# Weight parts of a fused attention and feed-forward kernel arrive where their low halves will stand, two per turn

## What is computed

```python
def _attn_ref(q, k, v, p):                  # q,k,v: 8 batches, 8 heads, 576 x 64; p: 32 x 64 per head
    p_packed = sm_attn(p, k, v)             # softmax(p k^T / 8) v
    return sm_attn(q, p_packed, p_packed)   # softmax(q pp^T / 8) pp

def _moe_ref(x, w_in, w_out, a, b):         # w_in 512 x 2048, w_out 2048 x 512
    h = x @ w_in
    P = a[0] + a[1] * h + a[2] * h * h + a[3] * h * h * h
    Q = 1.0 + np.abs(b[0]) * np.abs(h) + np.abs(b[1]) * h * h
    return (P / (Q + 1e-06)) @ w_out

def _moe2_ref(x, w_in, w_out, g_ln):        # 512 -> 1024 -> 512, softmax-weighted h, layer norm
    ...
```

## Time and profile before

| | us |
|---|---|
| median of 3 runs | 1235.49 |
| lowest and highest | 1233.49, 1236.66 |
| the profiled execution, its own time | 1235.92 |
| its span (first to last instruction) | 1234.1 |
| TensorE busy | 1180.6 (96%) |
| VectorE busy | 1045.4 (85%) |
| ScalarE busy | 832.8 (67%) |
| GpSimd busy | 437.5 (35%) |

### The profile page before, as it was taken

How to read it: one execution, slowest core, us unless ns; L and a number is a source line. 1 busy time by engine, 2 the same in 40 slices (tenths; PEclk the granted TensorE clock), 3 DMA queues, 4 the chain that set the end, 5 groups by cost and what they waited for, 6 DMA issues and landing times.

```text
span 1234.1 us, 25214 instructions
## 1 busy us (share of the span) xinstructions
PE 1180.6 (96%) x9824; PEld 1049.5 (85%) x9824; DVE 1045.4 (85%) x1621; ACT 832.8 (67%) x1302; POOL 437.5 (35%) x284
## 2 busy tenths in 40 slices
PE   6788887999999999999999999999999999999998
PEld 3455555999999999999999999997788888888887
DVE  3767778999999999999999999988677687776763
ACT  2456559888888888888888888754555454454543
POOL 1333322334343343333433334354434344353300
PEclk8889889999999999999999999999999999999999
DMA  8779975321202212012121121121121121111211
GB/s 286 226 265 348 333 272 217 105 81 38 81 28 64 81 38 80 29 62 81 43 75 37 55 80 37 54 88 44 43 54 49 36 58 43 51 47 38 60 26 35
DMA packets 70758, 116.25 MB, mean 94 GB/s; under 512 B 9728, under 2 KB 40448, under 8 KB 70656
## 3 DMA queue, kind: packets, MB, share of 16 engines
q1 hardware_dynamic: 70656, 114.85, 28.8%
HBM read 74.46 MB, written 40.37 MB: 93 GB/s over the span
## 4 chain that ended last, share of the span: by engine, by line
PE 90%; DVE 5%; issue 3%; ACT 1%; DMA 1%; POOL 0%; SPq 0%; ACTq 0%; DVEq 0%
PE ps_y L73 11%; PE ps_y L75 11%; PE ps_y L74 11%; PE ps_h L73 6%; PE ps_h L75 6%; PE ps_h L74 6%; PE ps_o L73 5%; PE ps_o L75 5%; PE ps_o L74 5%; PE ps_h L1394 4%; PE ps_h L1395 4%; PE ps_h L1396 4%; PE ps_s L381 3%; PE ps_s L394 3%; PE ps_t L1419 2%
## 5 line engine op out<-in xcount | busy, mean ns | idle before, releaser
L1018 POOL TENSOR_TENSOR den<-den,h_abs 128x576 f32<-128x576 f32 x128 | 222.3, 1737 | 401.6 <-ACT den L971 401.6
L73 PE MATMUL ps_y<-g_hi,wout_hi 128*128 128x288 f32 x1024 | 303.6, 297 | 0.0
L74 PE MATMUL ps_y<-g_lo,wout_hi 128*128 128x288 f32 x1024 | 302.6, 295 | 0.0
L75 PE MATMUL ps_y<-g_hi,wout_lo 128*128 128x288 f32 x1024 | 301.6, 295 | 0.0
L75 PEld LDWEIGHTS ps_y<-g_hi,wout_lo 128*128 128x128 f32 x1024 | 193.0, 188 | 0.0
L74 PEld LDWEIGHTS ps_y<-g_lo,wout_hi 128*128 128x128 f32 x1024 | 192.3, 188 | 0.0
L73 PEld LDWEIGHTS ps_y<-g_hi,wout_hi 128*128 128x128 f32 x1024 | 192.1, 188 | 0.3 <-ACT wp_out L530 0.2
L73 PE MATMUL ps_h<-x_hi,wp_hi 128*128 128x288 f32 x512 | 152.3, 298 | 1.3 <-DVE wp_lo L1033 0.8
L74 PE MATMUL ps_h<-x_lo,wp_hi 128*128 128x288 f32 x512 | 151.3, 295 | 0.0
L75 PE MATMUL ps_h<-x_hi,wp_lo 128*128 128x288 f32 x512 | 150.8, 295 | 0.0
L965 ACT ACTIVATE h_abs<-ps_h 128x576 f32<-128x576 f32 x128 | 83.3, 651 | 82.5 <-PE ps_h L75 82.3
(11 more groups left out here) (164 smaller groups left out, 2594.7 us busy)
## 6 DMA issues: line engine op xcount, KB each, us to landing
wp_scratch<-wp_out SPq DMA_DIRECT2D x32, 512.0 KB, 5.3
wp_lo<-wp_scratch SPq DMA_DIRECT2D x32, 512.0 KB, 4.1
k_main<-in_k SPq DMA_DIRECT2D x16, 576.0 KB, 6.7
q_main<-in_q SPq DMA_DIRECT2D x16, 576.0 KB, 6.0
v_main<-in_v SPq DMA_DIRECT2D x16, 576.0 KB, 5.5
y_scratch<-y_out SPq DMA_DIRECT2D x16, 576.0 KB, 3.4
y_lo<-y_scratch SPq DMA_DIRECT2D x36, 256.0 KB, 3.2
out<-result SPq DMA_DIRECT2D x144, 64.0 KB, 1.7
```

The costliest lines, as they stand in the source:

```text
L73: pe.matmul(out, lh, rh, start=first, stop=False)
L74: pe.matmul(out, lh, rl, start=False, stop=False)
L75: return pe.matmul(out, ll, rh, start=False, stop=last)
L1018: pool.tensor_tensor(den[s % 3][:, :, :], den[s % 3][:, :, :], h_abs[:, :, :], ALU.mult)\
```

## The change

There is no `w_stage` any more. Part n is loaded into the very bytes of `win_lo` or `wout_lo` where its low half will be written (`w_raw`), so ScalarE reads it there and GpSimd subtracts in place. The space of `w_stage` (4 KB of each partition) stays reserved. Loads are in another place of SyncE's order: part 0 at the start as before, and in turn i, i = 0 to 7, parts 2i+1 and 2i+2 (part 15 alone in turn 7) between the packed queries and the queries, without a wait for GpSimd. Part 15's load waits for the first high part, long done, since it counts on the same semaphore as part 0. The arrivals count on 8 semaphores in place of one. `second_block` no longer waits for the last low part. The order of work on TensorE, VectorE, ScalarE and GpSimd is the same; which part is split in which turn is too.

```diff
-    w_stage = sb("w_stage", [P, WI])
+    offset += 4 * WI
...
+    w_raw = [sbuf.at(f"w_raw1_{n}", [P, WI], sbuf.w_in + 32768 + 4 * WI * n) for n in range(PARTS)]
+    w_raw += [sbuf.at(f"w_raw1_{PARTS + n}", [P, WO, DM], sbuf.w_out + 32768 + 4 * WI * n) for n in range(PARTS)]
...
+    def w_loads(i):
+
+        return range(2 * i + 1, min(2 * i + 3, 2 * PARTS))
+
+    def w_arrival(n):
+
+
+        return w_in_sem[(n + 1) // 2 % PARTS], 16 if n == 0 else 32
...
     def load_w(sp, n):
-        stage, part = w_part(n, 0)
-        sp.dma_start(stage, part).then_inc(w_in_sem, 16)
+        if n == 2 * PARTS - 1:
+            sp.wait_ge(w_hi_done, 1)
+        sp.dma_start(w_arrived(n), w_part(n, 0)).then_inc(w_arrival(n)[0], 16)
...
-    def next_w(sp, n):
-        sp.wait_ge(w_lo_done, n)
-        load_w(sp, n)
...
                 load_p(sp, i + 2)
+                for n in w_loads(i):
+                    load_w(sp, n)
                 sp.wait_ge(qT_done, i + 1)
                 load_q(sp, i + 2)
             else:
                 first_chunk(sp)
-            if len(parts_at(i)) > 1:
-                next_w(sp, parts_at(i)[1])
             wait_for(sp, pack_done, i)
             load_v(sp, i + 1)
...
-            if parts_at(i + 1):
-                next_w(sp, parts_at(i + 1)[0])
...
         def weights_high(act, n):
-            act.wait_ge(w_in_sem, 16 * (n + 1))
-            stage, high = w_part(n, 1)
-            act.activation(high, stage, ACT.Copy).then_inc(w_hi_done, 1)
+            act.wait_ge(*w_arrival(n))
+            act.activation(w_part(n, 1), w_arrived(n), ACT.Copy).then_inc(w_hi_done, 1)
...
         def weights_low(pool, n):
-            stage, high = w_part(n, 1)
+            high, low = w_part(n, 1), w_part(n, 2)
             pool.wait_ge(w_hi_done, n + 1)
-            pool.tensor_tensor(w_part(n, 2)[1], stage, high.bitcast(F32), ALU.subtract).then_inc(w_lo_done, 1)
+            pool.tensor_tensor(low, w_arrived(n), high.bitcast(F32), ALU.subtract).then_inc(w_lo_done, 1)
...
     def second_block(sp):
         sp.wait_ge(attention["qT_done"], GROUPS)
-        sp.wait_ge(attention["w_lo_done"], GROUPS)
         load_block(sp, 0, 1)
```

More of the change, by code:

```diff
@@ L209, in attention_block @@
     p_in_sem = [sem(f"p_in_sem{i}") for i in range(2)]
-    w_in_sem = sem("w_in_sem")
+    w_in_sem = [sem(f"w_in_sem{n}") for n in range(PARTS)]
     w_hi_done = sem("w_hi_done")
@@ L258, in w_part, with w_arrived @@
         if n < PARTS:
-            return w_stage[:, :], (win_d, win_hi, win_lo)[which][:, m // 2, (m % 2) * WI:(m % 2 + 1) * WI]
-        return w_stage.rearrange("p (ft n) -> p ft n", ft=WO), \
-            (wout_d, wout_hi, wout_lo)[which][:, m * WO:(m + 1) * WO, :]
+            return (win_d, win_hi, win_lo)[which][:, m // 2, (m % 2) * WI:(m % 2 + 1) * WI]
+        return (wout_d, wout_hi, wout_lo)[which][:, m * WO:(m + 1) * WO, :]
+    def w_arrived(n):
+        return w_raw[n][:, :] if n < PARTS else w_raw[n][:, :, :]
+    def w_loads(i):
+        return range(2 * i + 1, min(2 * i + 3, 2 * PARTS))
+    def w_arrival(n):
+        return w_in_sem[(n + 1) // 2 % PARTS], 16 if n == 0 else 32
     def runs_of(a, i):
```

## The result

The changed kernel takes 1223.3 us (median of 8 runs, 1219.9 to 1225.9), the kernel before 1235.1 beside it (median of 8, 1229.2 to 1236.8). The ratio is 0.991, interval 0.989 to 0.993. The profiled execution of the changed kernel has a time of 1224.47 and a span of 1222.7, that of before 1235.92 and 1234.1. So the forecast of -1.4 us met a change of -11.5 us by the profiles and -11.8 by the medians.

The account below looks back on a forecast made before the run. The prediction took TensorE's own chain to bound the kernel, with the change's worth decided in attention. It summed -0.9 (turn 1) and -0.5 (later fetches) to -1.4 us against 1235.92, so 1234.5; the 8-in-10 range was 1228.5 to 1241.0.

Parts of the forecast that it names:

- Step 1: Compute engines: same instructions and bytes, so reading another SBUF address and subtracting in place was taken as 0.
- Step 2: ScalarE's waits for weight parts go away; only turn 1's counts, -0.9 us, the other five taken at nothing.
- Step 3: SyncE no longer waits 24.6 us for GpSimd; keys, queries and stores behind it go out earlier, worth 0.
- Step 4: DMA work moves, 0.52 MB per turn, from turns 8 to 13 to turns 0 to 5; direct worth 0.
- Step 5: Late instruction fetches stalling TensorE in `pack`: length hangs little on load, so turns 8 to 14 gain 0.5 us.
- Rival A: Attention turns 8 to 14: fetches wait behind queued data and get shorter, -6.0 us, 1229.9; chance 0.34.
- Rival B: Attention turns 0 to 5: fetch stalls grow, late turns gain nothing, +6.5 us, 1242.4; chance 0.18.
- Rival C: Turn 1: the weight part doesn't come earlier, 1235.4; chance included in the forecast's 0.42.

Follow-up runs that it names:

- e1: Changed kernel's in-place parts, but SyncE's load order and wait for GpSimd as in the kernel before; ratio to the kernel before 1.0003.
- e4: Kernel before without the loads of weight parts 10 to 15, all waits kept; ratio to the kernel before 0.9947.
- e8: Kernel before without the loads of keys, queries and values from group 4 on; ratio to the kernel before 0.9966.
- e11: Kernel before with keys and packed queries issued ahead of the job's stores, behind the weight load and its wait; ratio to the kernel before 1.0045.
- e16: In-place parts with the kernel before's order and waits, save parts 1, 6 and 7 loaded one or more turns earlier; ratio to the kernel before 0.9970.
- e3: Changed kernel plus an unread 512 KB load at the end of each of turns 8 to 13; ratio to the kernel before 0.9950.
- e5: Changed kernel with SyncE's old wait for GpSimd back at the turn's end, no weight load behind it; ratio to the kernel before 0.9919.
- e10: Changed kernel with keys and packed queries ahead of the job's stores from turn 6, and three parts per turn in turns 0 to 4; ratio to before 0.9938.
- e15: Changed kernel with keys and packed queries issued behind the values from turn 6 on; ratio to the kernel before 0.9962.
- e9: Changed kernel with keys and packed queries issued ahead of the last job's stores from turn 6 on; ratio to the kernel before 0.9965.
- e12: The changed kernel run once more with no edit; ratio to the kernel before 0.9915.
- e6: Changed kernel with one part per turn, a turn ahead of use, and the loads of parts 10 to 15 left out; ratio to the kernel before 0.9920.
- e7: Changed kernel with both weight loads moved to the turn's end, without a wait; ratio to the kernel before 0.9949.
- e2: Changed kernel with one part loaded per turn, a turn ahead of use, at the changed kernel's place; ratio to the kernel before 0.9941.

## Why the forecast was wrong, point by point

**What bounds the kernel, and where the gain must lie**: right. The stretch behind attention is 1019 us in both.

**Step 1, reading and subtracting in place is worth 0**: right (e1, 1.0003).

**Step 2, ScalarE's wait for parts, -0.9**: the mechanism was right, the term was mis-sized: it measured -3.7 to -6.2. I took turn 1 from one execution and set turn 6 to nothing, since TensorE showed no wait there. In e1, e4 and e8 the wait of TensorE for `packT` lies 4.1 to 6.0 us above the floor of 2.6, in e11 2.6 us; in the profile of before only 0.8. Early parts are worth 3.7 us (e16), at most the 6.2 of e3. I even named the price of the cover, 3.7 us, but gave it no weight. The load landed now just in time and now late: for part 7 ScalarE waited 0.56 us before, 1.63 in e4 and 4.44 in e1, so one trace could not size it.

**Step 3, SyncE's wait is worth 0**: right for the keys, queries and stores behind it (e5); its part in late weight loads belongs to step 2. Behind the first load of all, no engine waited for keys, queries or values in the changed kernel.

**Step 4, moved DMA work has no direct worth**: right as far as any instruction's semaphore goes, and the shares in turns 4, 5, 8 and 10 were 0.80, 0.84, 0.92 and 0.87 as against 0.85 foretold; turn 11's stayed at 0.99, since the shorter turn moves its bytes in less time.

**Step 5, the late stalls lose 0.5 us**: this is the step that failed. They went from 11.5 us to 5.6 and 4.4, the clock of turns 7 and 14 rose to 1.00, and the late loads are worth 4.9 us (e3) to 6.5 (e4) in time. I had averaged early and late stalls, found 1.8 and 1.9 us, and concluded that load hardly matters. The load in bytes alone indeed doesn't set the late ones (e8), but the mean mixed places at which data was queued with places at which it wasn't. With something in the pause the late stalls were 7.2 to 11.8 us in eight of nine kernels (e10 is the exception, 5.7), without it 3.5 to 6.9 in all seven. Turn 9 shows it best. Filled: 2.17 us before, 2.98 in e11, 3.06 in e15, 1.35 in e8, 1.20 in e3, 1.16 in e9, 0.84 in e1, 0.80 in e10, none in e16. Empty: none in the changed kernel, e12, e4, e5 and e6, 0.80 in e7 and e2. So it is a matter of means, 1.5 us against 0.2, and not a law for one place in one execution; and turn 9 is the turn in which it shows most, turns 8 and 11 hardly show it.

The rule of the Trainium skill (DMA: Bandwidth & Descriptors, "Queues, rings and completion order") by which a fetch would wait for one packet at most gave no change of the stalls. What the runs show is 4.9 to 6.5 us of time for six loads of 512 KB (e3, e4), and fetches that start 2 us later with 0.8 to 1.2 MB queued than with nothing, so as I applied it, with a packet too short to matter, the rule doesn't hold here. That half the bytes leave most of the stalls (e8) and that 608 KB in the wrong place bring some back (e9) says the same: what is queued at the moment of the fetch counts. The flat part above 1.2 MB would suit a wait for a bounded piece, but that was not settled.

**Rival A** (fetches wait behind queued data, -6.0, 1229.9) had the mechanism of the late half, fetches held up by queued data, its direction and nearly its size: e4's 0.53% is 6.5 us, where A had 4.8 + 2.1 less 1.8 for early stalls that didn't grow. It lacked the early half; with 3.7 to 6.2 for that, the two come to 10.2 to 12.7, beside the 11.5 measured. **Rival B** was wrong: the early stalls were 4.8 and 7.3 us against 7.2, with 0.80 and 0.84 of DMA share in turns 4 and 5. **Rival C** was wrong for turn 1 already: L433 started 1.1 us sooner, where I had said 0.9.

**The range** (1228.5 to 1241.0) ended 5.2 us above the median measured. It took half of rival A's stalls and no more than 0.9 for ScalarE, so both gains at full size lay outside it.

**What stays open**: whether a fetch waits for all that is queued or for a bounded piece; why e10 has few late stalls, and why its fetch of turn 8 started without delay with 1.3 MB queued; why e2 is not as fast as e6; and whether the early half has more in it than the waits in turns 1 and 6. That the filled pause makes the late half, and not a late load as such, rests on e2, e9, e11 and e15 and on the fetches' starts; no kernel differs from another by the pause alone without also moving something else. None of the variants beat the changed kernel.

## What to carry to other kernels

A load whose buffer comes free just in time lands now in time and now late: a wait that one execution doesn't show may cost 4 us in the next, so look for it by the distance between landing and use, over several executions, and issue the load early where the final place is free anyway. Where an engine stalls with no semaphore behind it, look whether an instruction packet lands just ahead of each restart. If so, ask what the data queue holds when the fetch is due, not how busy it is on average: six loads that TensorE never waited for cost 0.4 to 0.5%, and the stalls differ most in the turns whose fetch is due in the pause that they fill. An average over such stalls says little; compare place by place.

## What the runs showed of the hardware

- TensorE's instructions come in packets of 16 KB on a DMA queue of their own, and where one comes late TensorE stops: 157 gaps in 16 executions, all at 16 places of the program, each ending 1.0 to 1.6 us after such a packet. They are 0.2 to 3.7 us long, and the length at one place varies by 2 us and more between executions of one kernel (turn 8: 3.50 and 1.35).
- The packet starts late when data is queued as it is due: 0.3 us (median) after the earliest place with under 0.1 MB queued, 2.3 us with 0.8 to 1.2 MB. The mean DMA share doesn't tell it: 8.7 us of gaps from 83 to 176 us at a share of 0.54 (e8), 3.5 us at 0.91 where the six weight loads were gone but all other data kept (e4).
- Late turns with no gap, or one of 0.41, took 9.1 to 9.5 us (7, 10 and 14), with the DMA engines up to 1.01 busy at 378 GB/s and the granted clock at 1.00, its upper level, 2.4 GHz. Turn 8, with a gap of 3.50 us, took a further 1.9 us (14.61 - 9.20 - 3.50), with a clock of 0.84.
